# Attention and two expert layers: request order on GpSimd, halved last products, weights behind the second gather

## What is computed

```python
def _moe_ref(x, w_gate, w1, w2, capacity):
    logits = x @ w_gate
    expert_idx = np.argmax(logits, axis=1)
    ...
    h = np.maximum(np.einsum('ecd,edf->ecf', disp, w1), 0.0)
    y = np.einsum('ecf,efd->ecd', h, w2)
    ...
            out[i] = gate_w[i] * y[expert_idx[i], pos[i]]

def _moe2_ref(x, w_skip, w_gate, w1, w2):
    do_compute = x @ w_skip > 0
    out = x.copy()
    ...
        h = np.maximum(xc[mask] @ w1[e], 0.0)
        y[mask] = gate_w[mask, None] * (h @ w2[e])
    out[do_compute] = xc + y
```

## Time and profile before

| | us |
|---|---|
| median of three executions | 615.25 (614.92 to 615.62) |
| the profiled execution | 616.29 |
| its span | 614.50 |
| TensorE busy | 591.7 |
| VectorE (DVE) busy | 313.5 |
| ScalarE (ACT) busy | 266.3 |
| GpSimd (POOL) busy | 188.5 |

### The profile page before, as it was taken

How to read it: one execution, slowest core, us unless ns; L and a number is a source line. 1 busy time by engine, 2 the same in 40 slices (tenths; PEclk the granted TensorE clock), 3 DMA queues, 4 the chain that set the end, 5 groups by cost and what they waited for, 6 DMA issues and landing times.

```text
span 614.5 us, 12427 instructions
## 1 busy us (share of the span) xinstructions
PE 591.7 (96%) x3711; PEld 351.9 (57%) x3712; DVE 313.5 (51%) x659; ACT 266.3 (43%) x438; POOL 188.5 (31%) x164
## 2 busy tenths in 40 slices
PE   8899999999999999999999999999899999999992
PEld 7677787777777777777333333333594333333330
DVE  5457565757575766656353963955665220322220
ACT  4655565555565655620344444442102444444410
POOL 4785535444352800001011121122212122222222
PEclk9999999999999999999999999999989999999997
DMA  8979818171621062004999697762757789831111
GB/s 205 291 185 257 185 40 170 43 161 50 145 47 38 3 221 107 22 11 138 402 404 362 256 391 274 260 272 64 272 186 253 265 306 330 318 135 44 45 52 55
DMA packets 42637, 111.61 MB, mean 182 GB/s; under 512 B 16020, under 2 KB 16020, under 8 KB 41536
## 3 DMA queue, kind: packets, MB, share of 16 engines
q1 hardware_dynamic: 38528, 99.03, 50.8%
q0 software_dynamic: 4080, 12.22, 5.7%
HBM read 102.68 MB, written 12.06 MB: 187 GB/s over the span
## 4 chain that ended last, share of the span: by engine, by line
PE 88%; DVE 3%; issue 3%; DMA 2%; ACT 2%; POOLq 0%; DVEq 0%; POOL 0%; SPq 0%; ACTq 0%
PE psum L932 40%; PE psum L701 14%; PE psum L715 12%; PE psum L749 9%; PE psum L919 4%; PE psum L782 3%; PE psum L840 2%; PE psum L761 1%; PE psum L745 1%; DVE probs L1204 1%; ACT probs L1045 1%; PE psum L934 1%; DMA qraw<-in_q_dram 1%; DMA res<-moe_in,idx_r 1%; DMA xraw<-moe_in,rows_in 1%
## 5 line engine op out<-in xcount | busy, mean ns | idle before, releaser
L932 PE MATMUL psum<-w1ring,XT 128*64 x304 | 134.5, 595 | 0.8 <-issue 0.3
L932 PE MATMUL psum<-w2ring,HT 128*64 x320 | 133.7, 571 | 1.3 <-DVE wright L318 0.7
L934 PE MATMUL psum<-wright,XT 128*64 128x512 f32 x304 | 134.5, 595 | 0.0
L934 PE MATMUL psum<-wright,HT 128*64 128x512 f32 (+1 forms) x320 | 133.7, 571 | 0.0
L1204 DVE TENSOR_SCALAR_CACHE_REDUCE probs<-psum 128x1152 f32<-128x1152 f32 x72 | 97.6, 1357 | 62.5 <-PE psum L701 62.5
L1045 ACT ACTIVATE probs<-probs,nmax 128x1152 f32<-128x1152 f32 x72 | 90.7, 1260 | 45.6 <-DVE probs L1204 45.6
L701 PE MATMUL psum<-KT,QT 128*128 128x384 f32 x480 | 102.0, 350 | 2.7 <-DVE probs L1204 1.8
L932 PEld LDWEIGHTS psum<-w2ring,HT 128*64 128x64 f32 x320 | 43.7, 137 | 85.0 <-issue 83.0
L701 PEld LDWEIGHTS psum<-KT,QT 128*128 128x128 f32 x480 | 80.2, 188 | 14.7 <-issue 7.9
L932 PEld LDWEIGHTS psum<-w1ring,XT 128*64 128x64 f32 x304 | 40.1, 137 | 79.7 <-issue 79.7
L715 PE MATMUL psum<-ident,probs 128*128 128x128 f32 x648 | 82.0, 275 | 1.1 <-ACT probs L1045 0.6
(11 more groups left out here) (164 smaller groups left out, 636.7 us busy)
## 6 DMA issues: line engine op xcount, KB each, us to landing
w1ring<-in_moe_w_dram SPq DMA_DIRECT2D x64, 512.0 KB, 7.1
w2ring<-in_moe_w_dram SPq DMA_DIRECT2D x64, 512.0 KB, 7.4
qraw<-in_q_dram SPq DMA_DIRECT2D x30, 288.0 KB, 10.1
kraw<-in_k_dram SPq DMA_DIRECT2D x14, 576.0 KB, 9.0
V<-in_v_dram SPq DMA_DIRECT2D x8, 576.0 KB, 3.9
moe_in<-zero SPq DMA_DIRECT2D x9, 256.0 KB, 3.1
wnext<-in_next_w_dram SPq DMA_DIRECT2D x1, 2304.0 KB, 17.2
out_dram<-moe_in SPq DMA_DIRECT2D x1, 2304.0 KB, 9.4
```

Of the source, the lines that this page charges most:

```text
L932: pe.matmul(psum[0:GRAIN, b, 0:width], lhs[:, c * P:c * P + GRAIN], left, start=first, stop=last, skip_group_check=True)
L934: return pe.matmul(psum[GRAIN:P, b, 0:width], lhs[:, c * P + GRAIN:(c + 1) * P], wright[k][:, cols], start=first, stop=last, skip_group_ch ...
```

## The change

GpSimd's round t becomes: residual of t (layer 1), store of y of t-1, x of t+2. The last y product of layer 1 is done in halves as well, into two PSUM banks, and DVE adds the residual to each half when it is ready. ScalarE instead of DVE copies the turned y of layer 0's last tile. The last row of logits has a semaphore of its own, so DVE waits on a constant. SP waits for two gathers of x (32) instead of one (16) before its weights, in both layers. One filler less stands behind the count in either layer. TensorE reads the expert of tile 0 from memory before it turns tile 0.

```diff
@@ -197,7 +197,8 @@
         hot_ready, pos_ready, exp_ready, diff_ready = (sem(n) for n in ("hot_ready", "pos_ready", "exp_ready", "diff_ready"))
         tile_ready, inside_ready, kept_ready = sem("tile_ready"), sem("inside_ready"), sem("kept_ready")
         active_ready, ot_part = sem("active_ready"), sem("ot_part")
-        ylast_copied, y_half = sem("ylast_copied"), sem("y_half")
+        ylast_copied, last_logits = sem("ylast_copied"), sem("last_logits")
+        y_half_, orow_half = [sem(f"y_half_{m}") for m in range(2)], sem("orow_half")
         ids_ready, placed, gates_cut = sem("ids_ready"), sem("placed"), sem("gates_cut")
         rows_found, gates_found = sem("rows_found"), sem("gates_found")
         tables_ready, rows_in_ready, rows_ready = sem("tables_ready"), sem("rows_in_ready"), sem("rows_ready")
@@ -460,7 +461,7 @@
             attention_over(sp)
             sp.wait_ge(zeroed, NT * 16)
             sp.wait_ge(x_stored, 16 * 4 * H)
-            sp.wait_ge(x_loaded_[0], 16)
+            sp.wait_ge(x_loaded_[0], 32)
             load_matrix(SECOND, 0, 0)
             load_matrix(SECOND, 0, 1)
             load_matrix(FIRST, 0, 3)
@@ -489,7 +490,7 @@
             sp.wait_ge(y_stored_[0], rest * 16 + 32)
             sp.dma_start(out, x_dram[1]).then_inc(out_filled, 16)
             sp.wait_ge(tables_ready, 2)
-            sp.wait_ge(x_loaded_[1], 16)
+            sp.wait_ge(x_loaded_[1], 32)
             load_second(1, 2, 0, 7)
             middle_experts(1)
             for e in (6, 7):
@@ -633,18 +634,16 @@
                 def count_before(t):
 
                     if isinstance(t, int):
-                        return {0: 0, 1: 0, 2: 1 + m}[t]
-                    return t * (2 + m) - (3 + m)
-
-                def after(t, n):
-                    return count_before(t) + 1 + n
+                        return {0: 0, 1: m, 2: 1 + 2 * m}[t]
+                    return t * (2 + m) - 3
 
                 def step(t, first=False):
-                    if m == 1 and not first:
-                        load_residual(t - 1, after(t, 0))
-                    load_x(t + 2, after(t, 0 if first else m))
+                    count = count_before(t)
+                    if m == 1:
+                        load_residual(t, count + 1)
                     if not first:
-                        store_y(t - 1, after(t, m if isinstance(t, int) else m + 1))
+                        store_y(t - 1, count + (1 + m))
+                    load_x(t + 2, count + (2 + m))
 
                 n = ROUTED[m]
                 token = token_id if m == 0 else slot_token
@@ -667,13 +666,13 @@
                 with pool.Fori(2, NSLOT) as t:
                     with pool.If(t < rest + 2):
                         step(t)
-                done = rest * (2 + m) + (1 + m)
+                done = rest * (2 + m) + (1 + 2 * m)
                 if m == 0:
                     store_y(rest + 1, done + 1, last=True)
                     pool.wait_ge(y_stored, rest * 16 + 32)
                 else:
-                    load_residual(rest + 1, done + 1)
-                    store_y(rest + 1, done + 2)
+                    pool.wait_ge(orow_half, 1)
+                    store_y(rest + 1, done + 1)
                 pool.wait_ge(x_loaded, rest * 16 + 64)
                 settle()
 
@@ -884,7 +883,7 @@
                     for t in range(n):
                         mm = counted(whole, t, t + 1, n + 1)
                 mm.then_inc(pos_ready, 1)
-                keep_busy((14, 14)[m], HID_BANK + 1)
+                keep_busy((13, 13)[m], HID_BANK + 1)
 
                 pe.wait_ge(ids_ready, m + 1)
                 for t in range(n):
@@ -934,10 +933,14 @@
                     return pe.matmul(psum[GRAIN:P, b, 0:width], lhs[:, c * P + GRAIN:(c + 1) * P], wright[k][:, cols],
                                      start=first, stop=last, skip_group_check=True)
 
-                def hidden_product(t):
+                def hidden_place(t):
 
                     expert = left_expert(t)
-                    slot = pe.snap(ring_slot(FIRST, m, expert))
+                    return expert, pe.snap(ring_slot(FIRST, m, expert))
+
+                def hidden_product(t, place=None):
+
+                    expert, slot = place or hidden_place(t)
                     wait(pe, relu_ready, t)
                     for c in range(DC):
                         pe.wait_ge(w_loaded[FIRST][c], expert * 16 + (E * m + 1) * 16)
@@ -980,7 +983,7 @@
                             at = c * DM + half * 2 * P
                             mm = product(SECOND, HT, (Y_BANK, X_BANK)[half], c, slice(at, at + 2 * P), slot,
                                          c == 0, c == FC - 1, 2 * P)
-                        mm.then_inc((y_half, y_done)[half], 1)
+                        mm.then_inc((y_half_[m], y_done)[half], 1)
 
                 def turn_hidden(t):
                     pe.wait_ge(relu_ready, t + 1)
@@ -1007,8 +1010,8 @@
                                        start=(c == 0), stop=(c == DC - 1))
                     mm.then_inc(lg_done, 1)
 
-                def step(t, first=False):
-                    hidden_product(t)
+                def step(t, first=None):
+                    hidden_product(t, first)
                     if first:
                         pe.wait_ge(gates_found, m + 1)
                     else:
@@ -1018,9 +1021,10 @@
 
                 pe.wait_ge(tables_ready, m + 1)
                 rest = pe.value_load(tab_n[m][0:1, 0:1], min_val=0, max_val=NSLOT - 2)
+                own = hidden_place(0)
                 turn_x(0)
                 keep_busy(3, HID_BANK + 1)
-                step(0, first=True)
+                step(0, first=own)
                 step(1)
                 with pe.Fori(0, (NSLOT - 2) // GROUP) as g:
                     with pe.If(g * GROUP < rest):
@@ -1028,10 +1032,8 @@
                             t = pe.snap(g * GROUP + (i + 2))
                             with pe.If(t < rest + 2):
                                 step(t)
-                if m == 1:
-                    y_product(rest + 1)
-                else:
-                    last_y_product(rest + 1)
+                last_y_product(rest + 1)
+                if m == 0:
                     keep_busy(2, HID_BANK + 1)
                     turn_y()
                     keep_busy(2, HID_BANK + 1)
@@ -1185,10 +1187,14 @@
                 relu(rest + 1)
                 copy_hidden(rest + 1)
                 if m == 0:
-                    act.wait_ge(y_half, 1)
+                    act.wait_ge(y_half_[0], 1)
                     nc.scalar.copy(ylast[:, 0:2 * P], bank(Y_BANK, 2 * P)).then_inc(ylast_copied, 1)
                     act.wait_ge(y_done_[0], rest + (2 + START))
                     nc.scalar.copy(ylast[:, 2 * P:4 * P], bank(X_BANK, 2 * P)).then_inc(ylast_copied, 1)
+                    for i in range(2):
+                        half = slice(i * 2 * P, (i + 1) * 2 * P)
+                        act.wait_ge(y_turned, i + 1)
+                        nc.scalar.copy(yT[:, half], bank(YT_BANK + i)[:, half]).then_inc(yt_ready, 1)
 
 
         @block.vector
@@ -1411,7 +1417,7 @@
 
                 L = logits[:] if m == 0 else logits2[:, :, 0:E]
                 if m == 1:
-                    dve.wait_ge(lg_copied, dve.value_load(tab_n[0][:], min_val=0, max_val=NSLOT - 2) + 2)
+                    dve.wait_ge(last_logits, 1)
                     nc.vector.tensor_scalar(active[:], logits2[:, :, E], 0.0, 2.0 * E, ALU.is_gt, ALU.mult).then_inc(active_ready, 1)
 
                 reduce(of(r_max), L, ALU.max)
@@ -1518,16 +1524,18 @@
                     with dve.If(t < rest + 1):
                         step(t)
                 if m == 0:
-                    for i in range(2):
-                        half = slice(i * 2 * P, (i + 1) * 2 * P)
-                        dve.wait_ge(y_turned, i + 1)
-                        nc.vector.tensor_copy(yT[:, half], bank(YT_BANK + i)[:, half]).then_inc(yt_ready, 1)
                     at = bass.ds(rest + 1, 1)
                     dve.wait_ge(lg_done, 1)
                     nc.vector.tensor_copy(logits2[:, at, :].rearrange("p o c -> p (o c)"), bank(LG_BANK, E + 1)
-                                          ).then_inc(lg_copied, 1)
+                                          ).then_inc(last_logits, 1)
                 else:
-                    copy_y(m, rest + 1)
+                    dve.wait_ge(y_stored_[1], rest * 16 + 16)
+                    dve.wait_ge(res_loaded, rest * 16 + 32)
+                    dve.wait_ge(y_half_[1], 1)
+                    nc.vector.tensor_tensor(orow[:, 0:2 * P], bank(Y_BANK, 2 * P), res[:, 0:2 * P], ALU.add).then_inc(orow_half, 1)
+                    dve.wait_ge(y_done_[1], rest + (2 + START))
+                    nc.vector.tensor_tensor(orow[:, 2 * P:4 * P], bank(X_BANK, 2 * P), res[:, 2 * P:4 * P], ALU.add
+                                            ).then_inc(y_copied_[1], 1)
 
 
```

## The result

| | before | after |
|---|---|---|
| median of 20 runs each, us | 615.26 | 613.62 (611.61 to 616.68) |
| ratio | | 0.9975, 95% interval 0.9966 to 0.9984 |
| profiled execution, span | 616.29, 614.50 | 615.05, 612.3 |

The change gains 1.6 us, not 4.1: the time is 2.4 above the forecast of 611.2, near the upper end of its range. The profiled execution gains 2.2 us of span. Where they are, by four places of the trace (start of a first pass, before and after): last y product of layer 0 435.73 and 440.18, **4.45 lost**; first hidden product of layer 1 463.39 and 464.94, 2.9 gained; last product of layer 1 596.43 and 598.27, 0.3 lost; from there to the last store's issue 12.56 and 8.53, 4.0 gained. The first differs most from the forecast (2.7 lost), the third by 0.3.

A forecast was written before the change was run, and what follows sets the result against it. TensorE, busy 96% of the span, was taken as the bound, with time to gain only where it waits, runs slowly or has ended. 0.2 - 2.9 + 2.8 + 4.0 = 4.1 us off 615.25 gave 611.2, range 608.2 to 614.0.

The forecast's parts named there:

- the price of the hold: Layer 0: weights behind the second x start 4.5 us late, so TensorE's third product loses 2.9 us (bounds 0.8 to 4.5).
- The first rival: Layer 0's weight stream makes up its late start, in the dip at 320 to 332: loss 0.8, time 609.1; chance 0.17.
- The half-clock rival: New holes at 312 and 336, or the old one's rest, bring clock 0.50 for 3.4 us, costing 1.7: 612.8; chance 0.19.
- the sum of the gains: Gains over the kernel: 0.2 filler and early read, 2.8 between the layers, 4.0 at the end.
- Filler and earlier read: Before tile 0: one filler less gains 0.2 us in layer 0; reading the expert earlier gains 0.
- First stall at 312: Layer 0: late w1 of expert 3 delays XT, TensorE 1.4 us late at 312.2, inside the 2.9 lost at 336.
- Between the layers: From layer 0's last y to layer 1: ScalarE copies, constant wait and full clock gain 2.8 us; 1.5 if the clock falls.
- End: End of layer 1: early residual and last product in halves gain 4.0 us (bounds 3.6 to 4.4).
- Halving itself: Last product of layer 1: passes of half width end alike, cost 0.0.
- Layer 1 feels its own hold: Layer 1's fill at 529.88 comes late by the hold: 4.3 us lost, 615.5, no change; chance 0.05.
- x late in every crowded round: x, requested last, lands too late in six crowded rounds, costing 6 us: 617.2; chance 0.09.

The follow-up runs named there:

- experiment 1: Layer 0's hold (SP's wait for 32) removed from the changed kernel: 609.91 us; layer 1's removed: 615.09; both removed: 610.41; layer 0's added to the kernel before: 619.45.
- seven profiles: Profiles with layer 0's full hold and no filler in the hole: changed kernel, its repeat, four variants and the kernel before with the hold; TensorE waits 1.06 to 3.11 us.
- the repeated changed kernel: The changed kernel run once more, nothing altered: median 614.54 us, ratio 0.9984 (0.9971 to 0.9996) to the kernel before.
- the table: List of all follow-up kernels, variants of the changed kernel or the kernel before, with ratios to the kernel before: medians 609.80 to 619.45 us.

## Why the prediction was wrong

Two terms of the sum failed. Of the 2.5 us between the forecast gain of 4.1 and the measured 1.6, about 1.0 is the first and 1.5 the second.

**The first step that failed is the price of the hold: 2.9 forecast, 3.9 to 5.8 measured on the medians.** (3.9 and 4.5 in the changed kernel by its two ratios against the mean of the two of experiment 1 without layer 0's hold, 4.1 in the kernel before, 5.2 and 5.8 with either part.) Its mechanism was right. SP's first weight went out at 290.48 (forecast 290.9), the fill started at 336.47 (about 336), the product at 337.61 (337.35), and in this profile nothing was made up: 300 to 320 moved 417 GB/s and 320 to 332 moved 353, where it had been 413 and 340. The first rival is out but for a part in one other profile, that without layer 1's hold (SP 5.1 us late, the fill 3.3). One reading against that rival was wrong: 413 GB/s is not the most that 12 us moved before the change, 302 to 314 moved 421. What was missed is what follows a late stream. The half-clock rival, at 0.19, came true in three of seven profiles, for 1.3 us. In two others the late weights met a request for x and TensorE stood some 1.6 us more. And the third tile's product is late by 1.7 to 4.4 us, not always by 2.9, since the fill starts 3.3 to 6.0 us late behind the same start of SP. I had the price from one run of a chain of queues as if it were a constant, and had set the things on top as rivals of which one at most is true; each only ever adds.
The Trainium skill, TensorE: Matmul & The Clock Gate, Part 1, says that the check runs freely and isn't tied to the kernel; the seven profiles agree so far that the same hole was met in some and not in others: half clock after waits of 2.04, 2.78 and 3.11 us and none after 2.62, 2.70 and 2.95. I had argued from one wait of 0.84 us without a fall and one of 1.36 with one, and gave 0.19.

**The second is the sum of the gains, 7.0 forecast and 5.3 to 5.7 measured: the way from the profile to the median.** I took 4.1 us off the median, 615.25, but two of the stalls that the change removes were larger in the profiled execution, 616.29, than in most runs. The half clock between the layers cost it 0.8, and profiles of three kernels with the same wait there or a longer one (before with the hold, with the end, with the order) don't have it. And from the last product to the last store it took 12.56 us; four profiles of kernels with the old end took 11.98, 12.10, 11.45 and 11.44, with 8.53 in the changed one. So the end gives 2.9 to 4.0, not 3.6 to 4.4. The last product of layer 1 came 0.3 us later too, where nothing was forecast: from its first hidden product to its last product every profile with the part between the layers takes 133.3 to 133.5 us, every other 133.0 to 133.2. Of the rest, 0.1 to 0.8 lies outside the span: time less span has a median of 1.8 us in the kernel before and with the order alone, 2.0 with the end, 2.15 with the part between the layers, 1.9, 2.6 and 2.0 in the three kernels without layer 0's hold. The causes of these two are open.

**Point by point.** Filler and earlier read, 0.2: right (row products at 278.85 for 279.09). First stall at 312, 1.4: it was 0.2 late (312.41 for 312.23), and 0.2 early to 1.1 late in the other six profiles with the full hold; inside the second in any case. Between the layers 2.8: 2.9 in the profile, about 1 of it a loss that the other profiles lack. End 4.0: 4.0 in the profile, 2.9 at the least. Halving itself costs nothing: 6.75 us from first to last pass start (598.27 to 605.02), then 0.43 to the add. Layer 1 feels its own hold: no. x late in every crowded round: no, and with the weights on time the order costs nothing in layer 0; beside late weights one round was late in two profiles of seven. What the rest sums to: 5.5 of gains less 3.9 of the hold is the 1.6 that was measured.

**A better version.** The change without layer 0's hold beats both kernels: 609.91 us, ratio 0.9909 (0.9895 to 0.9923); with x ahead of y in layer 0 besides, 609.80.

## What to carry to other kernels

A stream that keeps its queue full for tens of microseconds should not be started later for a transfer that nobody waits for: here 4.8 us of standing queue cost 3.9 to 5.8 us of time, most of it 45 us later. Price such a hole with what rides on it, clock and the next request that meets the late traffic, since they add. And see first where the profiled run lies among the runs: savings read from its stalls are to be taken off its own time. Where two changes remove the same stall, or one that comes and goes, count it once.

## What was not expected of the hardware

- The clock falls in some runs and not in others at the same place, and the length of the wait does not decide it (2.04 us and half, 2.95 us and full). Both in the changed kernel and in the kernel before with the hold it fell 331.09 us after it had first risen (5.81 to 336.91, 7.05 to 338.14), though in the second the hole had ended 0.76 us before (337.38); in the third profile that fell, 334.51 us after (4.59 to 339.10), 0.22 us behind the hole.
- In six profiles a gather of 128 rows landed 3.4 to 3.9 us after its request where no weights stood ahead of it (281 to 288), mostly 6.3 to 8.5 behind weights whose requests went out before it or with it, and up to 10.5 in the thick of the late stream (313.87 in the repeated changed kernel).
- How far a kernel's runs spread can hang on one wait: the seven kernels of the table that lack the hold spread over 0.2 to 1.6 us of span (4 to 11 runs each), the six with the full hold and no filler over 2.0 to 4.9 (5 to 12 runs). The number of runs counts as well: the kernel before, which lacks the hold, spread over 1.9 to 3.1 us in five groups of 17 or 23 runs.
